# A fused attention and MoE kernel on Trainium2: constant products, five banks and a second state place in its first three steps

## The reference

```
for t in range(768):                       # per batch (4) and head (8), head_dim 48
    state = alpha[t][:, None] * state + outer(k[t], v[t])
    y[t]  = q[t] @ state
x   = y as 3072 tokens x 384
x   = (sigmoid(x @ w_gate) * (x @ w_val)) @ w_out       # 384 -> 1536 -> 384
out = sum over 4 experts of p_e * relu(x @ w1[e]) @ w2[e]   # 384 -> 1024 -> 384
```

## Time and profile before

| | |
|---|---|
| median of 3 runs | 1374.7 us (1374.53 to 1377.53) |
| profiled execution | 1375.34 us |
| its span, first to last instruction | 1373.5 us |
| TensorE busy | 97% of the span |
| VectorE, ScalarE, GpSimd busy | 63%, 54%, 70% |

### The profile page before, as it was taken

One profiled execution on the slowest core, in us unless ns is written; L12 is line 12 of the kernel. 1 busy time (PEld: TensorE's weight loads), 2 busy tenths in 40 slices (PEclk: granted clock), 3 DMA queues, 4 the chain that ended last, 5 costly groups with the idle time before them and its releaser, 6 DMA issues.

```text
span 1373.5 us, 33443 instructions
## 1 busy us (share of the span) xinstructions
PE 1335.8 (97%) x12962; PEld 1234.0 (90%) x12962; DVE 859.1 (63%) x1361; ACT 739.6 (54%) x1501; POOL 965.8 (70%) x924
## 2 busy tenths in 40 slices
PE   3899999999999999999999999999999999999999
PEld 2788999999999999998999999999989999999998
DVE  8775756556574756244757576666766666666666
ACT  5654646455464555346565655555755555555552
POOL 6575555545554657378888989887888777777772
PEclk9999999999999999999999999999999999999999
DMA  9413221312212212001101010101030111101001
GB/s 328 126 57 111 83 85 56 112 56 92 74 59 91 76 58 90 12 12 58 47 24 47 24 46 23 46 23 46 24 115 24 37 33 36 35 29 40 23 11 69
DMA packets 42425, 83.73 MB, mean 61 GB/s; under 512 B 5824, under 2 KB 31168, under 8 KB 42304
## 3 DMA queue, kind: packets, MB, share of 16 engines
q1 hardware_dynamic: 42304, 82.01, 18.9%
HBM read 77.28 MB, written 4.72 MB: 60 GB/s over the span
## 4 chain that ended last, share of the span: by engine, by line
PE 91%; DVE 4%; issue 2%; DMA 1%; POOL 1%; ACT 1%; SPq 0%; POOLq 0%; DVEq 0%; ACTq 0%
PE PS L909 29%; PE PS L898 24%; PE PS L793 21%; PE PS L803 11%; PE PS L730 2%; PE PS L763 1%; PE PS L759 1%; PE PS L742 1%; DVE KQ L1227 1%; DMA KQ<-in_qka 1%; PE PS L747 0%; PE PS L734 0%; PE PS L777 0%; DMA V<-in_v 0%; PE PS L772 0%
## 5 line engine op out<-in xcount | busy, mean ns | idle before, releaser
L1498 DVE SCALAR_TENSOR_TENSOR acc<-PS,prob,acc 128x384 f32<-128x384 f32 x360 | 221.9, 616 | 209.5 <-PE PS L909 209.5
L1004 ACT ACTIVATE QX<-KQ 48x256 f32<-48x256 f32 x288 | 120.7, 419 | 119.9 <-DVE KQ L1227 84.9
L1129 ACT ACTIVATE mixed<-PS 128x512 f32<-128x512 f32 x192 | 112.6, 589 | 89.8 <-PE PS L898 89.0
L1227 DVE TENSOR_TENSOR KQ<-KQ,TOT 112x512 f32<-112x512 f32 (+1 forms) x126 | 119.4, 968 | 31.5 <-PE PS L742 14.8
L1346 DVE TENSOR_TENSOR hid<-PS,hid 128x384 f32<-128x384 f32 x96 | 53.6, 558 | 123.7 <-PE PS L793 111.3
L1157 ACT ACTIVATE mixed<-mixed 128x512 f32<-128x512 f32 x192 | 118.3, 616 | 0.0
L1582 POOL TENSOR_TENSOR hs0l<-hid,hs0h 128x384 fp32r<-128x384 f32 x48 | 58.5, 1218 | 68.7 <-ACT hs0h L1023 68.7
L1582 POOL TENSOR_TENSOR hs1l<-hid,hs1h 128x384 fp32r<-128x384 f32 x48 | 57.2, 1192 | 68.1 <-ACT hs1h L1023 68.1
L1156 ACT ACTIVATE H_1h<-mixed 128x512 fp32r<-128x512 f32 x32 | 20.3, 634 | 130.5 <-DVE mixed L1472 130.5
L1549 POOL TENSOR_TENSOR row<-row 128x384 f32<-128x384 f32 x24 | 25.1, 1047 | 82.7 <-DMA V<-in_v 82.7
L1019 ACT ACTIVATE hid<-PS 128x384 f32<-128x384 f32 x96 | 47.2, 491 | 56.2 <-PE PS L793 52.5
(11 more groups left out here) (543 smaller groups left out, 4962.9 us busy)
## 6 DMA issues: line engine op xcount, KB each, us to landing
row<-in_rows SPq DMA_DIRECT2D x24, 768.0 KB, 4.3
KQ<-in_qka SPq DMA_DIRECT2D x24, 672.0 KB, 4.8
rawA<-in_w SPq DMA_DIRECT2D x32, 384.0 KB, 3.1
rawB<-in_w SPq DMA_DIRECT2D x32, 384.0 KB, 3.3
V<-in_v SPq DMA_DIRECT2D x24, 384.0 KB, 4.9
out_y<-acc SPq DMA_DIRECT2D x24, 192.0 KB, 2.5
raw<-in_w_gate SPq DMA_DIRECT2D x3, 768.0 KB, 14.6
raw<-in_w_val SPq DMA_DIRECT2D x3, 768.0 KB, 13.4
```

Source lines behind the costliest of these rows:

```text
L1004: done = nc.scalar.activation(QX[p][rows, :, g, :].rearrange("d a (n t) -> d a n t", t=2 << level), right, ACT.Copy)
L1129: nc.scalar.activation(mixed[:, COPIED[g], :], PS[:, hidden_banks[HIDDEN[g]], :], ACT.Copy).then_inc(copied, 1)
L1227: dve.tensor_tensor(x, x, y, ALU.mult).then_inc(kq_ready[p], 1)
L1498: dve.scalar_tensor_tensor(out=to, in0=result, scalar=weight, in1=to, op0=ALU.mult, op1=ALU.add).then_inc(acc_ready, 1)
```

## The change

1. `FIRST_BANKS`: the 30 tasks of the first steps rotate over five banks, 3 to 7, not three; VectorE clears five, before QX, and TensorE waits for that (`banks_clear`) and for POOL's memsets before its first task. Behind the first steps it waits until banks 3 and 4 have been copied out.
2. `WARM` and `keep_warm`: before some level tasks TensorE multiplies a constant tile by itself, 32 products of 128 x 128 x 128 in fp32, written to the task's bank and then overwritten.
3. Levels 0 to 3 of the first steps use two lanes of 64 rows, not four of 32.
4. `ST1`: the state after step 1 has a place of its own, so that scaling it doesn't wait for readers of the old one; `scale_state` for step 1 stands behind `STATE` 0.
5. Another order of the last tasks of `FIRST`; the rectangle of (2, 4) goes to ACT, that of (1, 5) moves behind (2, 4); ACT's rectangles of step 2's levels 3 and 4 move behind `TRK` 0 and `TRK` 1.
6. The first gate and value groups are whole groups: gate before `STATE` 2, value behind it. ACT waits for `state_done` before its sigmoid; VectorE's preparation and ACT's spread of step 3 stand behind the value group.
7. Weight pieces move in the lists of ACT, VectorE and POOL; POOL's high copies are functions of their own.
8. In every tile the `STATE` task stands at the end of its slot, behind `PREP`.

```
-            if level == LEVELS + 1:
-                tasks.append((STATE, j, 0))
         slots[at(n)] += tasks
+    for n in range(LEVELS - AHEAD + 1, 4 * STEPS_T, 4):
+        slots[at(n)].append((STATE, (n + AHEAD - LEVELS - 1) // 4, 0))
...
-        FIRST += [(STATE, 0, 0), (YOUT, 0, 0), (TRK, 1, 0)]
-FIRST += [(YOUT, 1, 0), (STATE, 1, 0), (TRX, 0, 0), (TRX, 1, 0), (YOUT, 2, 0), (TRK, 2, 0), (TRX, 2, 0), (STATE, 2, 0)]
+        FIRST += [(STATE, 0, 0), (TRK, 1, 0), (YOUT, 0, 0)]
+FIRST += [(STATE, 1, 0), (YOUT, 1, 0), (TRX, 0, 0), (YOUT, 2, 0), (TRX, 1, 0), (TRX, 2, 0), (TRK, 2, 0), (STATE, 2, 0)]
+FIRST_BANKS = (0, 1, 2, -2, -1)
+WARM = {(LVL, 0, 0): 9, (LVL, 0, 1): 7, (LVL, 0, 2): 5, (LVL, 0, 3): 3, (LVL, 1, 2): 2, (LVL, 2, 1): 2, (LVL, 0, 4): 1, (LVL, 1, 3): 1,
+        (LVL, 2, 2): 1, (LVL, 0, 5): 1}
-FIRST_KEPT = {(LVL, 0, 5): (0, 5), (LVL, 2, 3): (1, 4), (LVL, 1, 5): (1, 5), (LVL, 2, 4): (2, 4)}
+FIRST_KEPT = {(LVL, 0, 5): (0, 5), (LVL, 2, 3): (1, 4), (LVL, 2, 4): (1, 5)}
...
+            def keep_warm(bank, idle, n):
+                for _ in range(n):
+                    pe.matmul(bank[:, 0:C], idle[:], idle[:], start=True, stop=True)
...
+                if base == 0:
+                    keep_warm(bank, AT[STEPS_T - 1][:, 0, :] if level < 3 and j == 0 else ones, WARM.get((kind, j, level), 0))
-                            lanes = LANES if level < TILED else lanes_of(i, sc)
+                            lanes = lanes_of(i, sc)
...
+            pe.wait_ge(at_clear, 1)
+            pe.wait_ge(banks_clear, 1)
             for t in FIRST:
+                if t == (LVL, 0, 3):
+                    pe.wait_ge(mask_in, 16)
...
+                if t == (STATE, STEPS_T - 1, 0):
+                    group(0, 0, "gate", 0)
                 task(0, 0, *t)
-            first_part("gate", STEPS_T - 1, STEPS_T)
-            first_part("value", STEPS_T - 1, STEPS_T)
+            group(0, 0, "value", 0)
+            for bank in (-2, -1):
+                last = [t for n, t in enumerate(FIRST) if first_bank(n) == bank][-1]
+                wait_count(pe, *kept(last[0], 0, *last[1:]))
...
-            high_after = {(LVL, 0, 2): (0,), (TRX, 1, 0): (3, 4), (TRX, 2, 0): (5,)}
+            high_after = {(LVL, 1, 2): (0,), (TRX, 1, 0): (3, 4), (TRX, 2, 0): (5,)}
-                if t == (LVL, STEPS_T - 1, MASKED):
+                if t in ((LVL, STEPS_T - 1, MASKED), (LVL, STEPS_T - 1, MASKED + 1)):
                     next_columns(0, 0, *t)
-                    task(0, 0, *t)
                     continue
                 task(0, 0, *t)
+                if t == (TRK, 0, 0):
+                    task(0, 0, LVL, STEPS_T - 1, MASKED)
+                if t == (TRK, 1, 0):
+                    task(0, 0, LVL, STEPS_T - 1, MASKED + 1)
...
+            act.wait_ge(state_done, per_state(0, STEPS_T - 1, 1))
             group(0, 0, "gate", 0)
+            group(0, 0, "value", 0)
             spread_heads(0, STEPS_T, 0)
-            group(0, 0, "value", 0)
...
-            parts_after = {(YOUT, 2, 0): ((3, 0), (3, 1)), (TRX, 2, 0): ((3, 2), (4, 0), (4, 1))}
+            parts_after = {(YOUT, 2, 0): ((3, 0), (3, 1)), (STATE, 2, 0): ((3, 2), (4, 0))}
...
+                if t == (STATE, 0, 0):
+                    scale_state(0, 1)
+            group(0, 0, "value", 0)
             prepare(0, STEPS_T, 0)
             prepare(0, STEPS_T, 1)
-            group(0, 0, "value", 0)
-            parts = [(4, 2)] + [(5, k) for k in range(THIRD)]
+            parts = [(4, 1), (4, 2)] + [(5, k) for k in range(THIRD)]
...
             near_products(0, 2)
+            high_raw1(1)
+            near_terms(0, 2)
             low_raw1(1)
-            near_terms(0, 2)
+            high_raw1(2)
             low_raw1(2)
...
-            tile(0, 0, between={5 + at + n - 6: (lambda n=n, k=k: low_part1(n, k)) for at, (n, k) in enumerate(parts)})
+            tile(0, 0, between={at: (lambda n=n, k=k: low_part1(n, k)) for at, (n, k) in zip((3, 4, 5, 6, 7, 10, 11, 12, 13, 14), parts)})
```

More of the change, by code:

```diff
@@ L164, in in_use, with first_bank @@
     return kind not in (TRK, STATE) or sc % CHUNKS < CHUNKS - 1
+def first_bank(n):
+    return FIRST_BANKS[n % len(FIRST_BANKS)] if n < len(FIRST) else n - len(FIRST)
 def bank_of(task, base):
     if base == 0:
-        return (FIRST + LEAD).index(task) % ATT_BANKS
+        return first_bank((FIRST + LEAD).index(task))
     if task in SEQUENCE:
@@ L181, in before_in_bank @@
     if base == 0:
-        n = (FIRST + LEAD).index(task) - ATT_BANKS
-        return (FIRST + LEAD)[n] if n >= 0 else None
+        n = (FIRST + LEAD).index(task)
+        same = [m for m in range(n) if first_bank(m) == first_bank(n)]
+        return (FIRST + LEAD)[same[-1]] if same else None
     n = SEQUENCE.index(task) - ATT_BANKS
@@ L359, in attention_moe_program @@
         WV = [sb(f"WV{c}", [P, KD, F1], F32R) for c in "hl"]
+        ST1 = nc.alloc_sbuf_tensor_at("ST1", [P, PAIRS, 2 * D], F32, offset=top[0] - PAIRS * 2 * D * 4)
         last_third = [top[0] + (n * FC1 + FC1 - THIRD) * DM * 4 for n in range(2)]
@@ L436, in attention_moe_program @@
         at_clear = sem("at_clear")
+        banks_clear = sem("banks_clear")
         mask_in = sem("mask_in")
@@ L531, in ynat_of, with state_of @@
             return ynat1 if is_first(i, sc) and sc == 1 else ynat
+        def state_of(i, sc):
+            return ST1 if is_first(i, sc) and sc == 1 else ST
         def row_of(i, sc):
@@ L709, in state_rows @@
                 return slice(HB * g, HB * g + LW), slice(HB * g + LW, HB * g + D)
+            ones = mask[:].rearrange("s l r -> s (l r)")[:, 0:C]
+            def keep_warm(bank, idle, n):
+                for _ in range(n):
+                    pe.matmul(bank[:, 0:C], idle[:], idle[:], start=True, stop=True)
             def task(i, base, kind, j, level):
@@ L1324, in task @@
                     if chunk:
-                        if not base:
+                        if not base and sc == 2:
                             scale_state(i, sc)
                         dve.wait_ge(state_scaled, per_scaled(i, sc))
+                    to = state_of(i, sc)
                     for w, rows in heads:
@@ L1330, in task @@
                         if chunk:
-                            done = dve.tensor_tensor(ST[rows, :, mine], ST[rows, :, mine], new[rows, :, mine], ALU.add)
+                            done = dve.tensor_tensor(to[rows, :, mine], to[rows, :, mine], new[rows, :, mine], ALU.add)
                         else:
@@ L1363, in low_part1 @@
                     done.then_inc(raw_split_dve, 1)
+            nc.vector.memset(PS[:, att_bank0 + min(FIRST_BANKS):att_bank0 + ATT_BANKS, :], 0.0).then_inc(banks_clear, 1)
             for p in range(3):
                 nc.vector.memset(QX[p][:], 0.0)
-            nc.vector.memset(PS[:, att_bank0:att_bank0 + ATT_BANKS, :], 0.0)
             prepare(0, 0, 0)
@@ L1599, in low_raw1 @@
                 else:
-                    pool.wait_ge(raw1_in[n], 16)
-                    nc.gpsimd.tensor_copy(high, raw_piece(n)).then_inc(own_high, 1)
                     pool.wait_ge(own_high, n)
```

28 lines of the change are left out of this document (8 added, 20 removed).

## The result

| | before | after |
|---|---|---|
| median of 7 runs each | 1374.74 us (1374.27 to 1377.53) | 1380.31 us (1378.91 to 1382.09) |
| profiled execution | 1375.34 | 1379.49 |
| its span | 1373.5 | 1377.7 |

The ratio is 1.0035, 95% interval 1.0024 to 1.0047: slower, by 3.3 to 6.5 us, under half a per cent. The forecast was 1370.1, its range ended at 1373.6.

What follows compares the result with a forecast made beforehand. TensorE's own work bounds the kernel after 53.2 us, VectorE paces it before. Gains of 3.4 (earlier first output group) and 1.2 (swap), 4.6 in all, gave 1370.7 from the profiled execution, 1370.1 against the median; range 1367.8 to 1373.6.

Steps and rivals of the forecast that it cites:

- Where a part of it goes again: Between the third y and first output group, ACT's weight copies delay x to 47.45 us; net gain 3.4 us.
- the cost of 0 for the constant products: First steps: the 32 products fit into TensorE's waits and cost 0, at worst 1 us; they likely raise the clock before 20 us.
- first state: End of the first steps' state: 37.2 us instead of 40.35, from three closed waits and one rectangle less, 3.5 us.
- the section on the clock: Start: 1.2 GHz until about 40 us, then 2.4, despite the column; otherwise about 1.5 us from faster level products is lost.
- rival (c): Start: too few products, clock low until about 39 us; about 2.5 us lost, 1372.6, or 1373.6 with products in the way; chance 0.13.
- Low clock later: 0: Behind the first stage: one low-clock stretch counted, as before, at the new 3.3 us hole by the gate group: 0.
- Rival (a): The clock falls at both places, the new hole and the 77 us stretch: 1371.7 us; chance 0.20.
- The swap, 1.2: Every tile: STATE behind PREP shortens TensorE's waits at 96.19 and 115.55 us, 0.53 + 0.72 = 1.2 us; bounds 0 to 1.6.
- The marker: First output group, 59.31 us in the kernel before, taken as where TensorE runs on, so its earlier start counts as gain.
- the forecast's 3.4: First output group at 55.9 us instead of 59.3: a gain of 3.4 us.
- Rival (d): Late instructions while DMA engines are full, in the third y and gate group; two bare stops give 1376.6 us; chance 0.07.
- a hole with issue behind 40 us: Sign that the forecast is wrong: a TensorE hole with "issue" as releaser behind 40 us.

Runs made afterwards that it cites:

- POOL's order of before: Changed kernel with ACT's first weight copy early and POOL's low part of the value weights ahead of step 2's near terms, both as before: 1376.30 us, ratio 1.0006.
- Parts behind the state: Changed kernel with VectorE's low parts (3,0) and (3,1) behind STATE 2 instead of YOUT 2: 1378.29 us, ratio 1.0015.
- No constant products: Changed kernel without its 32 constant products, nothing else changed: 1375.73 us, ratio 1.0003.
- the two with parts behind the state: Changed kernel with VectorE's parts (3,0) and (3,1) behind STATE 2: with the 32 products 1378.29 us, without products 1374.32 us.
- the last one: Kernel without products and with weight copies behind the copies of x, given the change's 32 constant products back: 1375.69 us, ratio 1.0001.
- Weights behind x: Changed kernel without constant products, all weight parts of ACT and VectorE behind x, eight of VectorE's in the first tile: 1372.42 us, ratio 0.9977.
- 54 and 56: Changed kernel with more constant products: 26 instead of 4 between 27 and 38 us, 1376.44 us; 24 more ahead of the first tile's gate group, 1375.82 us.
- The swap alone: Kernel before with only the STATE task put behind PREP in its slot in every tile: 1375.76 us, ratio 1.0000.
- All weights in the tile: Kernel without products, copies behind x, with all ten of VectorE's low parts in the first tile and POOL's at their old places: 1372.89 us, ratio 0.9981.
- before with products: Kernel before with only the constant products and the waits and memset order they need: 1375.62 us, ratio 1.0001.

## Why the prediction was wrong

**The step that failed is "Where a part of it goes again".** It has x complete at 47.45; it was at 52.43, since VectorE's two weight parts, which the sum leaves out there, collided with POOL's last low part. The second step that failed is the cost of 0 for the constant products.

| place | forecast | measured | off by |
|---|---|---|---|
| first state | 37.2 | 39.25 | 2.05 |
| last y of step 2 over | 42.65 | 44.3 | 1.65 |
| gate group starts | 47.5 | 52.58 | 5.1 |
| gate group to multiply | 4.2 | 6.7 | 2.5 |
| multiply to first output group | 4.2 | 4.2 | 0 |

1. *x complete.* I counted ACT's two copies rightly: x's last high part ended at 48.65, forecast 46.9, late by what it inherited. Behind it I gave VectorE's low part 0.5 us; x was complete 3.78 us behind it. The two parts that my sum names, ahead of the multiply, are those behind `STATE` 2. The two behind `YOUT` 2, which stand ahead of the low parts of x, have no term. Alone they cost next to nothing beside ACT's copies: without the collision x was complete 0.6 behind ACT. They cost 4.56 because POOL was in its last low part. By my own times it would have been there too, from 44.8 to 48.3, when ACT's first piece set the two parts free near 45; I didn't lay the two beside each other. That POOL ended at 50.95 made it no better. It was late by ACT's moved copy and by its own new order together: with the copy early alone its last part still began at 47.46, with both undone at 43.91. Undoing the collision ("POOL's order of before") or the order on VectorE ("Parts behind the state") gave 3 us at the gate group.
2. *First state.* The two stops with "issue" at 22 and 30 us did go, as forecast, and so did over half of the 1.29. In their place stand 0.33 + 0.60 + 0.54 for level products and 0.65 for POOL. I credited the waits at their full length and named ACT as late next; it was POOL. From the second inputs to the first state the change saves 1.0 us (31.2 to 30.2), not 3.15. It isn't the clock: this length is the same at the low and the high one, so the 1.5 us that the section on the clock hangs on faster level products aren't there, and neither is what rival (c) adds for slow ones.
3. *Constant products cost 0.* Wrong: 4.6, 4.0 and 3.3 us by the medians of the three pairs with 32 and without (after and "No constant products"; the two with parts behind the state; the last one and "Weights behind x"), 4.4, 2.8 and 3.3 by the ratios. They did what they say: clock up at 7 us, not near 39. But it fell again at 27.4. Up to the gate group they cost nothing, as forecast. Behind the first output group the traces of the three pairs differ by 3.1, 5.7 and 5.4 us, of which "issue" stops are 1.2, 3.6 and 3.7, and one low stretch more is 1.7 in the first and the third. That is one profiled execution each. Why 32 products cost 3 to 4 us, 54 and 56 next to nothing, and 32 in the kernel before nothing, stays open.
4. *Low clock later: 0.* I had weighed the hole against a wait of 1.81 and counted one stretch. The hole of 6.44 brought one that covered gate group, state and half of the value group. Of the 2.5 us in the row "gate group to multiply" 1.7 are the clock (6.7 against 5.0 with products in the hole). Most of the rest is VectorE, whose state and two parts put the multiply 2.6 us behind the state product, where I had 2.0. Rival (a) priced the clock at 1.65 for a shorter hole; its mechanism was right, and I gave it 0.20.
5. *The swap, 1.2.* By its median the swap alone gives 0 ± 1.2 us, which neither shows the 1.2 nor rules it out. The waits in after's trace don't decide it either, since its TensorE comes 5 us late. The tenth sigmoid tells more: in the three kernels with the swap whose TensorE isn't late it stands at 114.50, 114.51 and 114.60 ("The swap alone", "Weights behind x", "All weights in the tile"), in the two without it at 115.43 and 115.87 (before, and before with products); the last two of the three have other edits besides. At the sixth, 30 us earlier, they stood anywhere from 81.6 to 85.6. So these traces put this point some 0.9 us forward with the swap, though the waits are still there.
6. *The marker.* "From there TensorE runs on" fails for an early start. "Weights behind x" and "All weights in the tile" had gained 2.1 and 2.5 us at the first sigmoid; at 115 us they were 0.9 and 0.8 ahead, no more than the swap's run, which had gained nothing at the first but had no low stretch at 77 us. By these traces the forecast's 3.4 would not have lasted through that tile. The median of "Weights behind x" is 3.3 us under that of the swap all the same; where that gain lies, the traces don't show. A late start isn't given back in the same way: 4.3 late there, 3.9 at 115.
7. *Rival (d)*, slower through late instructions, had the right sign and wanted two bare stops behind 40 us. There are three, 2.6 us in all, but at other places than I said. And the kernel before has two there already, 1.1 us in all, which I hadn't looked for, so neither the rival's count nor my sign "a hole with issue behind 40 us" tells the two kernels apart. It is a part at most.

## What to carry to other kernels

When a step moves, lay the forecast times of POOL's long operations beside VectorE's operations with two SBUF inputs: two parts that took 1.3 us together took 4.6 in the collision. Compare early times of two traces from the landing of the inputs on and not from the start; a "gain" of 1.1 us was nothing else. Products that only keep the clock up bought nothing in a stage that VectorE paces, and they are instructions too; they are to be timed by medians, with none, some and more of them. And a wait that disappears in a slower kernel has not been won: look for it in a run of the one edit alone.

## What was not expected of the hardware

- TensorE stopped for instructions 1.2 to 1.5 us beyond the end of the packet, with the DMA engines idle (share 0.00 in the stop before 546.95) as well as full (1.37 and 1.35 in the two stops of the first stage). Full DMA engines, which had seemed the reason, aren't needed for a stop.
- The clock fell at 27.4 us, behind a time in which TensorE was working between waits of 0.4 to 1.1 us, and stayed low until 37.6 although TensorE was busy for 9.13 of the 10 us from 27.5. In the kernel before with products it stayed low from 19 to 31 us at 12.00 of 12. So in these two traces work at the low level did not bring the rise at once.
